# Sums of squares per head: from a VectorE reduction to ScalarE's accumulator, with the mean and epsilon inside the square root

## What is computed

```python
def _attn_ref(q, k, v, g_norm):            # q, k, v: 8 batches, 8 heads, 576 tokens, 64 wide
    kv = np.einsum('bhsd,bhse->bhde', k, v)
    out = np.einsum('bhsd,bhde->bhse', q, kv)
    rms = np.sqrt(np.mean(out * out, axis=-1, keepdims=True) + 1e-06)
    return (out / rms * g_norm).astype(np.float32)

def _moe_ref(x, w_ch1, w_ch2):             # x: 8 x 576 x 512
    X = np.fft.fft(np.fft.fft(x, axis=1), axis=2)
    u = x + np.real(X).astype(np.float32)
    mu = np.mean(u, axis=-1, keepdims=True)
    var = np.mean((u - mu) ** 2, axis=-1, keepdims=True)
    un = (u - mu) / np.sqrt(var + 1e-06)
    return (u + np.maximum(un @ w_ch1, 0.0) @ w_ch2).astype(np.float32)

def _moe2_ref(x, U, V, w_ch1, w_ch2):
    u = x + ((x.transpose(0, 2, 1) @ U @ V).transpose(0, 2, 1))
    return (u + np.maximum(u @ w_ch1, 0.0) @ w_ch2).astype(np.float32)
```

## Time and profile before

| | before |
|---|---|
| median of 3 executions | 1965.79 us (1965.09 to 1966.41) |
| span of the profiled execution | 1964.7 us |
| PE busy | 1905.0 us (97%) |
| DVE busy | 640.9 us (33%) |
| ACT busy | 359.1 us (18%) |
| POOL busy | 140.6 us (7%) |

### The profile page before, as it was taken

The page is one execution under the profiler, slowest core; times in us unless marked ns, Lnnn a source line. Parts: engine busy times, 40 slices in busy tenths (PEclk is TensorE's granted clock), DMA queues, the critical chain, the costliest instruction groups (busy, mean ns, idle before and its releaser), DMA issues.

```text
span 1964.7 us, 24175 instructions
## 1 busy us (share of the span) xinstructions
PE 1905.0 (97%) x9764; PEld 1677.6 (85%) x9764; DVE 640.9 (33%) x1126; ACT 359.1 (18%) x784; POOL 140.6 (7%) x124
## 2 busy tenths in 40 slices
PE   5988799999999999999999999999999999999999
PEld 4777589999999999999988888888988888888988
DVE  4899962222222222222224321221222221221221
ACT  1333331111111111111123211211111111211111
POOL 1566530000000000000000000000000000000000
PEclk8999899999999999999999999999999999999999
DMA  8445230000000000000213100010000000000000
GB/s 298 163 157 168 95 120 33 1 32 32 31 1 32 32 0 32 32 32 0 80 58 107 65 33 17 17 34 7 27 33 1 33 33 17 17 17 1 17 17 16
DMA packets 23138, 94.96 MB, mean 48 GB/s; under 512 B 4833, under 2 KB 7265, under 8 KB 20130
## 3 DMA queue, kind: packets, MB, share of 16 engines
q1 hardware_dynamic: 23074, 94.01, 14.0%
HBM read 65.69 MB, written 28.31 MB: 48 GB/s over the span
## 4 chain that ended last, share of the span: by engine, by line
PE 88%; DVE 6%; DMA 1%; issue 1%; SPq 1%; POOL 1%; DVEq 0%; ACT 0%; POOLq 0%
PE bank L476 14%; PE bank L478 14%; PE bank L463 14%; PE bank L462 14%; PE bank L464 14%; PE bank L477 14%; PE bank L454 2%; DVE eo_sb L817 1%; DVE eo_sb L815 1%; DMA q_sb<-q_t 1%; PE bank L531 1%; POOL x_sb L1038 1%; DVE ss_sb L790 1%; SPq L209 1%; DVE x_sb L803 0%
## 5 line engine op out<-in xcount | busy, mean ns | idle before, releaser
L891 DVE SCALAR_TENSOR_TENSOR h_lo<-bank,h_hi 128x384 fp32r<-128x384 f32 x384 | 214.0, 557 | 1212.5 <-ACT h_hi L699 1212.5
L464 PE MATMUL bank<-at_hi,w_lo 128*128 128x384 f32 x1536 | 514.7, 335 | 2.1 <-issue 2.1
L462 PE MATMUL bank<-at_hi,w_hi 128*128 128x384 f32 x1536 | 515.0, 335 | 1.3 <-issue 1.3
L463 PE MATMUL bank<-at_lo,w_hi 128*128 128x384 f32 x1536 | 515.9, 336 | 0.0
L476 PE MATMUL bank<-w_hi,h_hi 128*128 128x512 f32 x1152 | 463.7, 403 | 0.0
L478 PE MATMUL bank<-w_hi,h_lo 128*128 128x512 f32 x1152 | 456.0, 396 | 0.0
L477 PE MATMUL bank<-w_lo,h_hi 128*128 128x512 f32 x1152 | 453.9, 394 | 0.0
L699 ACT ACTIVATE h_hi<-bank 128x384 fp32r<-128x384 f32 x384 | 189.2, 493 | 1369.2 <-PE bank L464 1369.2
L462 PEld LDWEIGHTS bank<-at_hi,w_hi 128*128 128x128 f32 x1536 | 288.4, 188 | 17.3 <-issue 2.1
L463 PEld LDWEIGHTS bank<-at_lo,w_hi 128*128 128x128 f32 x1536 | 288.1, 188 | 15.0
L464 PEld LDWEIGHTS bank<-at_hi,w_lo 128*128 128x128 f32 x1536 | 288.4, 188 | 2.7 <-issue 2.7
(11 more groups left out here) (84 smaller groups left out, 970.3 us busy)
## 6 DMA issues: line engine op xcount, KB each, us to landing
q_sb<-q_t SPq DMA_DIRECT2D x8, 1152.0 KB, 5.2
u_dram<-x_sb SPq DMA_DIRECT2D x24, 384.0 KB, 3.1
u_sb<-u_dram SPq DMA_DIRECT2D x12, 768.0 KB, 4.2
x_dram<-u_sb SPq DMA_DIRECT2D x12, 768.0 KB, 3.3
x_sb<-x_dram SPq DMA_DIRECT2D x12, 768.0 KB, 5.1
out<-u_sb SPq DMA_DIRECT2D x12, 768.0 KB, 3.3
k_sb<-k_main SPq DMA_DIRECT2D x7, 1024.0 KB, 5.2
v_sb<-v_main SPq DMA_DIRECT2D x7, 1024.0 KB, 7.6
```

The costliest lines, as they stand in the source:

```text
L462: nc.tensor.matmul(ps[:, 0:TILE], w1_hi4[:, f, d, :], at_hi[:, d, :], start=(d == 0), stop=False)
L463: nc.tensor.matmul(ps[:, 0:TILE], w1_hi4[:, f, d, :], at_lo[:, d, :], start=False, stop=False)
L464: last = nc.tensor.matmul(ps[:, 0:TILE], w1_lo4[:, f, d, :], at_hi[:, d, :], start=False, stop=(d == ND - 1))
L891: nc.vector.scalar_tensor_tensor(h_lo[:, f % 2, :], hid_ps[f % 2][:, 0:TILE], 0.0, h_hi[:, f % 2, :].bitcast(F32), ALU.max, ALU.subtract). ...
```

## The change

ScalarE squares one head (96 x 64) at a time and writes the sum of each head straight to its column of `ss_sb` through the accumulator output: 16 instructions for a group instead of 2. The reduction and the mean-and-epsilon instruction leave VectorE, and the buffer `ms_sb` goes. The square root reads `ss_sb` with a scale of 1/64 and a bias taken from a small tile `eps_sb`, which VectorE fills once. `root` now waits for `squared` of its own engine and for `inverted`, so that the reciprocal has read `rms_sb` before it is overwritten. SyncE's wait on `summed` becomes one on `squared`.

```diff
-    ms_sb = at("ms_sb", a0 + 79808, [PT, 2, 2 * H])
+    eps_sb = at("eps_sb", a0 + 79808, [PT, 1])
...
-            sp.wait_ge(summed, NT * B)
+            sp.wait_ge(squared, NT * B)
...
             def square(b, g, first):
                 act.wait_ge(att_done, 6 * b + 2 * g + 2)
-                if g == 0 and not first:
-                    act.wait_ge(summed, NT * b)
-                if g == 2:
-                    act.wait_ge(summed, NT * b + 1)
                 for m in range(2):
-                    nc.scalar.activation(sq_sb[:, g % 2, m, :], att_ps[2 * (g % 2) + m][0:PT, :],
-                                         ACT.Square).then_inc(squared, 1)
-
-            def root(b, g):
-                act.wait_ge(meaned, NT * b + g + 1)
-                nc.scalar.activation(rms_sb[:, g % 2, :], ms_sb[:, g % 2, :], ACT.Sqrt).then_inc(rooted, 1)
+                    for h in range(H):
+                        cols = slice(HD * h, HD * (h + 1))
+                        last = nc.scalar.activation(sq_sb[:, g % 2, m, cols], att_ps[2 * (g % 2) + m][0:PT, cols], ACT.Square,
+                                                    accum_out=ss_sb[:, g % 2, H * m + h:H * m + h + 1])
+                last.then_inc(squared, 1)
+
+            def root(b, g, first=False):
+                act.wait_ge(squared, NT * b + g + 1)
+                if first and g == 0:
+                    act.wait_ge(eps_set, 1)
+                if not first or g == 2:
+                    act.wait_ge(inverted, NT * b + (0, -1, 1)[g])
+                nc.scalar.activation(rms_sb[:, g % 2, :], ss_sb[:, g % 2, :], ACT.Sqrt, bias=eps_sb[:, :],
+                                     scale=1.0 / HD).then_inc(rooted, 1)
...
             nc.vector.memset(warm_sb[:, :], 0.0).then_inc(warm_zeroed, 1)
+            nc.vector.memset(eps_sb[:, :], EPS).then_inc(eps_set, 1)
             nc.vector.memset(kv_sb[:, :, :], 0.0).then_inc(kv_zeroed, 1)
-
-            def sums(b, g):
-
-                dve.wait_ge(squared, 2 * (NT * b + g + 1))
-                nc.vector.tensor_reduce(ss_sb[:, g % 2, :], sq_sb[:, g % 2, :, :].rearrange("p m (h e) -> p (m h) e", h=H),
-                                        AX.X, ALU.add).then_inc(summed, 1)
-                dve.wait_ge(summed, NT * b + g + 1)
-                nc.vector.tensor_scalar(ms_sb[:, g % 2, :], ss_sb[:, g % 2, :], 1.0 / HD, EPS, ALU.mult, ALU.add).then_inc(meaned, 1)
...
             def phase1_step(b, first):
-                sums(b, 0)
-                sums(b, 1)
                 normalise(b, 0, not first)
                 normalise(b, 1, not first)
                 fold(b, 0, False)
-                sums(b, 2)
                 normalise(b, 2, not first)
```

More of the change, by code:

```diff
@@ L154, in build_program @@
         kv_summed, kv_copied = sem("kv_summed"), sem("kv_copied")
-        att_done, squared, summed, meaned = sem("att_done"), sem("squared"), sem("summed"), sem("meaned")
+        att_done, squared, eps_set = sem("att_done"), sem("squared"), sem("eps_set")
         rooted, inverted, scaled, x_ready = sem("rooted"), sem("inverted"), sem("scaled"), sem("x_ready")
@@ L672, in _ @@
             square(0, 1, True)
-            root(0, 0)
-            root(0, 1)
+            root(0, 0, True)
+            root(0, 1, True)
             copy_kv(1)
             square(0, 2, True)
-            root(0, 2)
+            root(0, 2, True)
             phase1_step(1, True, True)
@@ L867, in phase1_step @@
                     split_lo(0, w1_raw, w1_hi, w1_lo, 0)
-            sums(0, 0)
             normalise(0, 0, False)
-            sums(0, 1)
             normalise(0, 1, False)
             fold(0, 0, True)
-            sums(0, 2)
             normalise(0, 2, False)
```

## The result

| | before | after |
|---|---|---|
| median of the runs | 1966.06 us (1965.09 to 1966.41) | 1992.01 us (1986.94 to 1993.33) |
| profiled execution, span | 1964.7 us | 1988.9 us |
| first up-product of the tiles (L462) | 257.94 us | 283.07 us |

The changed kernel takes 1.0131 times as long, 95% interval 1.0116 to 1.0145. The direction was forecast and the time lies inside the range, but the forecast of 1972 us missed by 20 us. All of the loss is in the first phase: L462 starts 25.1 us later, and from there to the end the two profiled executions differ by 1.0 us (1706.8 and 1705.8).

The account below looks back on a forecast made before the run. Each first-phase step was taken as a ring through VectorE. Steady steps -1.5, step 1 +1.7 and clock falls +7.5 gave +7.7 us on the profiled 1964.7, 1973.5 for the median, stated as 1972 us; range 1956 to 2022.

Parts of the forecast that it names:

- The bound and the place: First phase, before 258 us: VectorE bounds the steps; only group 2's removed reduction counts, at most 1.69 us a step.
- The price of a head: ScalarE, c: time from one 64-column square to the next, accumulator output included; taken as 0.213 us.
- The root's bias: ScalarE's square root: a bias from a tile adds 0.10 us per root; root's start to next copy 0.22 us.
- The ring formula: Steady step: group 2's reciprocal comes at 191.88 + 48c against 202.35; at c = 0.213 a gain of 0.25 us.
- TensorE's own way round: Steady step: copies at 191.40 instead of 189.88, so L414 ends at 208.65, just within the new L425 at 208.72.
- the part without the clock: First phase: six steady steps -1.5 us, step 1 +1.7 us, batch 0 nothing; together +0.2 us.
- The growing pause: TensorE between L388's end and L392: idle time grows from 1.39 to 2.9 us in each of six steps.
- The price of the falls: TensorE's clock, from the pause before L392: three falls in six steps at 2.5 us each, +7.5 us.
- The price is low: ScalarE heads, c from 0.11 to 0.18: VectorE stays the bound, no clock falls, 1956 to 1959 us; chance 0.20.
- The clock holds: TensorE pause before L392, c near 0.21: stays in the tolerated range, 1963 to 1968 us; chance 0.19.
- each output waits for its square: ScalarE heads, c from 0.28 to 0.39: clock falls every time, about 2005 to 2041 us; chance 0.25.
- the forecast's own case: First phase, c near 0.21 with some clock falls: from 1967 to 1982 us; chance 0.36.

Follow-up runs that it names:

- experiment 3: Changed kernel with the 16 squares a group kept but no accumulator output, sums a constant 1.0: 1952.6 us, ratio 0.9936 to the kernel before.
- experiment 5: Kernel before with group 2 alone summed by the accumulator, and scale and bias in all roots: 1954.4 us, ratio 0.9946 to the kernel before.
- experiment 7: Kernel before with its squares and reductions, only mean and epsilon moved into the root's scale and bias: 1963.91 us, ratio 0.9993.
- Experiment 2: Changed kernel plus four unread TensorE products in the pause before L392, steps 1 to 7: 1960.41 us, ratio 0.9975 to the kernel before.
- experiment 4: Kernel before plus one extra ScalarE copy of 1024 columns ahead of the copies of slots 0 and 1: 1970.87 us, ratio 1.0034.
- experiment 6: Kernel before with only groups 0 and 1 summed by the accumulator, mean and epsilon in all roots: 1987.42 us, ratio 1.0119.

## Why the prediction was right or wrong

**The bound and the place: right.** Nothing after the first phase moved. Experiments 3 and 5 split the change just as the reading of the earlier trace rows had it: a step is 25.86 us with all reductions gone (3) and with only that of group 2 gone (5). So the removal ahead of groups 0 and 1 is worth nothing, since the product waits for the store (1.18 us in experiment 5), and the removal at group 2 is worth its 1.69 us a step.

**The price of a head: right in kind, 9% too high.** 0.196 us measured, 0.213 taken. The square was 0.107 for 0.106; the read 0.09 for 0.107. The row that I took for the read, a short instruction without a PSUM source, was the right neighbour. Of the rules cited, the one that an op with an accumulator output is two instructions, which the Trainium skill states for VectorE ("VectorE: DVE Perf Modes", section "Two Vector instructions with no wait between them"), holds here for ScalarE too, as the 384 ACTIVATION_READ_ACCUMULATOR show. The estimate of 0.146 us for a square, worked out from the figures of "ScalarE: Activation LUTs" in the Trainium skill, section "What ACT_TABLE_LOAD costs", is not what was measured: 0.107 in experiment 3, so the interpolation between rows was the better guide.

**The root's bias: right.** 306 against 215 ns in experiment 7, 0.09 for 0.10 us; root to copy 0.20 us for 0.22.

**The ring formula: right, if the clock is added.** At c = 0.196 the squares-to-reciprocal time of 7.52 + 48c is 16.93 us. In the step shown it is 222.38 - 203.40 = 18.98. Of the 2.05 us between them, 1.84 lie from the copies to the squares of group 2 (218.69 - 209.89 = 8.80, against 6.96): 1.69 are the slow L392, and 0.15 the copies, which took 0.84 us for 0.69. Without a fall the formula gives 201.29 for 202.35, a gain of 1.06 us a step, and not the 0.25 written down. TensorE's own way round allows less: the copies start 0.97 us later than before, so L414 ends at 208.10, and L425 can gain 0.87. Six times 0.87 less 1.2 for step 1 makes the part without the clock -4 us instead of +0.2. Experiment 2 has 0.73 a step, and its first up-product starts 3.2 us earlier, its filling included. (Its spans differ by 5.9, but 2.7 of that lie behind the first phase.)

**The growing pause: right in kind.** 2.44 us for 2.9, the difference being 32 heads at 0.017 us less. Step 1 was late by about what was said: from the first square to L392 it is 7.08 us (47.64 and 54.72), against 5.05 before and 7.48 forecast.

**The price of the falls: this is the step that failed.** The term was "three falls in six steps: +7.5 us", each 2.5. Measured are seven falls, in seven steps, and 31.6 us of TensorE's busy time. The mechanism was right, and this term of the sum was four times too small. It has two errors.
- *The count.* I read the earlier trace rows as two ends of a scale, 2.31 us held and 3.39 lost, and put 2.9 between them. By that reading 2.44 us would have been nearly safe, and the clock fell every time. Experiments 4, 6 and 7 show that there is no such scale: it fell with 1.65, 1.75 and 2.36 us, and with 2.34 it did both. Something other than the length of the pause has a part in it. Two rows were taken for a rule.
- *The price of one.* I capped it at the 6.2 us of work between L392 and the end of group 2's attention, and at the 2.3 to 3.1 us that this would lose. A long fall goes on for 13.6 us, through L392, L401, the attention and into L342, and costs 6.5. The estimate came from one fall behind the last step, of which it took the last 6.7 us, from the start of L388. That fall had begun at 230.5 us and lasted 17.1 us, for 6.2 of which TensorE stood still. Four of the seven falls of after were long ones, and TensorE worked through them.

**The rivals.** "The price is low" (0.20) had the price nearly right: c = 0.196 is below its 0.20, where it was said to decide. But its consequence, that no clock falls, did not come. The threshold in c was drawn from the ring, and the clock had its own. "The clock holds" and "each output waits for its square" did not occur; that the latter's low end (2005) is only 13 us off says nothing for it, since its cause was a head of 0.28 us. That the measured time lies inside the stated range is in part luck: the forecast's own case ended at 1982, and the range above that was there for this rival.

**What would show it.** Start to start 0.21: 0.196. VectorE's wait at group 2 of about 1 us: 2.44, of which 1.84 are the slow L392 and copies; the other 0.6 is what the ring formula gives at 0.196 (201.29 - 200.66). The clock at 0.50 in stretches: yes. Product of group 0 released by ScalarE: yes, by way of the reciprocal (210.16 and 210.73). After 258 us nothing: yes.

**Open.** Which pattern of pauses makes the clock fall is not settled. In the steps of after, the 2.44 us at L392 is TensorE's only wait; in the steps of experiment 4 with a held clock there is also one at L425, and there is none in those that follow a fall. But in experiment 7 the clock fell in a wait at L425. Nor do the runs say why long and short falls alternate in after. The steps do so with them: L388 starts at 82.09, 110.58, 143.51, 172.00, 204.94 and 233.43, which are 28.5 and 32.9 us in turn. In after and in experiment 6 a fall that began inside the pause lasted about 13.6 us and one that began behind it 3.4, in 14 of 14 steps. Elsewhere this does not hold: the fall of 10.2 us in experiment 4 began 1.8 us behind the start of its L392, and the one of 3.4 us in experiment 7 inside its pause.

## What to carry to other kernels

Before you lengthen an engine's run, look at what the others do behind it: here ScalarE's heads were cheap enough to win, and the TensorE pause behind them was not. Move a sum to the accumulator only where the separate reduction is on the ring (group 2), keep it where a DMA hides it anyway, and let copies that TensorE waits for go ahead of the long row. When the time moves and the instruction counts do not, compare TensorE's busy time first: it shows in one subtraction what the slow clock added, and a few matmuls into an idle bank show in one run whether it is the cause.

## What the runs showed of the hardware

- An accumulator output of ScalarE is an instruction of its own, ACTIVATION_READ_ACCUMULATOR; it adds 0.09 us to a square of 0.107, whatever its record's length. The records of a row of 32 grow from 0.22 to 0.36 us, while the spacing stays at 0.196: the mean of a group (267 ns) is not what one costs.
- An fp32 matmul is two instructions on TensorE here: eight products of 289 columns gave 16 records and took 3.9 us, 0.49 each.
- The clock of TensorE fell to 1.2 GHz in or up to 1.8 us behind pauses of 1.65 (experiment 6), 1.75, 2.34 (experiment 4), 2.36 (experiment 7) and 2.44 us (after). It held through others of 2.00 and 2.34 (experiment 4), 2.29 (experiment 7) and 2.31 us (before). It stayed down for 3.4, 10.2 or 13.6 us with TensorE busy again.
